# Top-32 attention with a routed feed-forward: selecting the last tile alone, a lighter mask, and earlier routing hops

## The chip, the cores and the metric

The kernel runs on one core of one Trainium2 chip. The metric is the device time of one execution in microseconds (us). TensorE (PE), VectorE (DVE), ScalarE (ACT), GpSimd (POOL) and SyncE (SP) each run their own instructions in order and meet through semaphores.

## The reference

Attention on q, k, v of 4 batches x 8 heads x 576 positions x 64, in which each query keeps only its 32 largest scores; the result, as 2304 tokens of 512 features, goes through a mixture of 8 experts with one expert for each token.

```
scores = q @ k.T / 8
kth    = 32nd largest of each row
attn   = softmax(where(scores >= kth, scores, -1e9))
x      = attn @ v                      # heads joined: 4 x 576 x 512
logits = x @ w_gate; local = sigmoid(x @ w_local)
e      = argmax(logits) if s == 0 or local < 0.5 else e of the token before
out    = softmax(logits)[e] * (relu(x @ w1[e]) @ w2[e])
```

## The kernel before

**Tiles and groups.** A unit is a pair of batches and a head; its 2 x 576 query rows make 9 tiles of 128 rows by 576 scores. All 16 units give 144 tiles. A round (`r`, 8 of them) handles two units in 6 groups (`k`) of 3 tiles (`j`). Rounds 1 to 3 are a hardware loop on each engine. Round 4 (`ROUND0`) is written out. Rounds 5 to 7 are written out on PE, ACT and POOL and are a hardware loop on DVE.

**The work on a group.** PE makes the scores of a tile and ACT copies them to `s_sb`, a ring of 9 slots (L760), two groups ahead. DVE finds the 32 largest in four passes of 8 (`largest`, L978 MAX8, L986 MATCH_REPLACE8 between the passes): 21 large instructions a group. The three tiles take turns, so that no instruction waits for the one just ahead. POOL then masks each tile in two passes: `(s < 32nd) * -1e9` into `p_sb` (L1277), and `p + s` (L1280). ACT takes the exponential and the row sum (L767), PE transposes (`turn`, L403), ACT copies the transposed tile (`take_pT`, L775), PE multiplies by v (`values`, L432), ACT copies (`take_oT`, L783), PE turns the group back and multiplies by the gate weights (`turn_back`, L444), ACT scales (`normalise`, L789, L797) and POOL adds the logits (`add_logits`, L1223, L1227). POOL also makes `nmax` (`biases`, L1261) and guards the row sums (`guard_sums`, L1216), which DVE inverts (`reciprocals`, L951).

**What sets the order.** Each engine's order is written out by hand. `step` on PE and ACT handles group `k`, with `values`, `take_oT` and `normalise` of the group before it; `ahead` makes the scores of the group after next. `slot` places parts of the early work at two places in a step.

**Early work.** After round 3 the first half of the tokens is complete. `early_routes` on PE and DVE works out, in hops placed in groups 1 to 4 of round 4, which token goes where. Then 29 parts (`early_parts`: a first transpose, and four parts for each of 7 row tiles) run one expert tile each for 7 experts, in slots of the following 19 groups; POOL gathers and scatters rows (`early_moves`).

**The last group.** After the loop DVE masks the three tiles itself (L1088, L1091), ACT takes three exponentials, and PE runs `turn`, `values(k-1)`, two `turn`s, `turn_back(k-1)`, `values`, `turn_back`. Then DVE routes the second half of the tokens (`choose`, L1005, and what follows), while PE fills its waits with the eighth early tile (`early_first`, L514; `early_second`, L522). PE's `code_rows` (L451) stand behind three quarters of one such product. The last stage, from 773 us on, is 15 expert tiles bound by PE (L681, L686).

## Time and profile before

| | us |
|---|---|
| median of 3 runs (lowest, highest) | 1013.66 (1013.32, 1015.21) |
| the profiled execution: its own time | 1011.88 |
| its span, first to last instruction | 1010.0 |
| busy: PE, DVE, ACT, POOL | 791.0, 762.0, 419.4, 613.7 |

Busy times are sums over the span; matmuls are pipelined, so a busy PE is not PE at its peak. The attention stage runs from about 20 to 747 us, the second routing to 773 us, the experts to the end. Line numbers are those of the kernel before.

### The profile page before, as it was taken

To read this page: it belongs to the slowest core of one execution; us is meant where nothing else is said; L and a number is where in the kernel's file an instruction comes from. 1 tells how busy PE (TensorE), PEld (TensorE's weight loads), DVE (VectorE), ACT (ScalarE), POOL (GpSimd) and SP (SyncE) were. 2 spreads that over 40 slices of the span, in tenths; PEclk is the share of its full clock that TensorE was granted. 3 is DMA by queue.
4 is the path that set the end of the run, shared out by engine and by line. 5 is a ranking of instruction groups with operands and counts; after the bars stand their busy time and mean duration, and the time that the engine had idled before them with its cause. 6 is when DMAs were issued, how large, how long until landed. Compare 5 with 4: busy or idle time off the path is not lost.

```text
span 1010.0 us, 16010 instructions
## 1 busy us (share of the span) xinstructions
PE 791.0 (78%) x3938; PEld 445.9 (44%) x3939; DVE 762.0 (75%) x1624; ACT 419.4 (42%) x914; POOL 613.7 (61%) x557
## 2 busy tenths in 40 slices
PE   2566666766766766567998889878888999999996
PEld 1343433434433443354554545545454444444442
DVE  5999999999999999899999999999944111111110
ACT  2445555544545555434565565656540111111111
POOL 0878887787878788568888888888812111101111
PEclk7667686676667577657999999999989999999998
DMA  3081001010101104010146145254135155454500
GB/s 122 1 352 65 20 31 49 2 48 13 36 13 35 48 0 142 1 48 22 60 178 235 55 183 219 81 205 184 57 146 188 51 190 208 189 195 162 232 22 27
DMA packets 17498, 103.98 MB, mean 103 GB/s; under 512 B 2638, under 2 KB 5198, under 8 KB 13328
## 3 DMA queue, kind: packets, MB, share of 16 engines
q1 hardware_dynamic: 10560, 57.68, 15.3%
q10 hardware_dynamic: 3024, 34.21, 8.6%
q0 software_dynamic: 3840, 11.28, 3.2%
q8 instruction: 25, 0.41, 0.2%
q14 instruction: 49, 0.40, 0.1%
HBM read 93.72 MB, written 10.75 MB: 103 GB/s over the span
## 4 chain that ended last, share of the span: by engine, by line
DVE 35%; PE 29%; issue 27%; POOL 3%; ACT 2%; DVEq 2%; DMA 1%; ACTq 0%; POOLq 0%
DVE top L978 19%; DVE work L986 13%; PE ps L681 10%; PE ps L686 10%; POOL p_sb L1277 2%; DVEq L200 2%; PE ps L522 1%; PE ps L403 1%; PE ps L670 1%; PE ps L432 1%; PE ps L514 1%; DMA wg_sb<-in_wg 1%; POOL p_sb L1280 1%; PE ps L662 1%; ACT p_sb L767 1%
## 5 line engine op out<-in xcount | busy, mean ns | idle before, releaser
L1277 POOL TENSOR_SCALAR p_sb<-s_sb,top 128x576 f32<-128x576 f32 x141 | 314.5, 2231 | 92.4 <-DVE top L978 89.2
L978 DVE MAX8 top<-work 128x8 f32<-128x576 f32 x432 | 302.4, 775 | 0.0
L403 PE MATMUL ps<-id_sb,p_sb 128*128 128x128 f32 x720 | 134.6, 331 | 184.6 <-ACT p_sb L767 184.6
L1280 POOL TENSOR_TENSOR p_sb<-p_sb,s_sb 128x576 f32<-128x576 f32 x141 | 198.6, 1409 | 26.2 <-POOL p_sb L1277 25.4
L986 DVE MATCH_REPLACE8 work<-top,work 128x576 f32<-128x576 f32 x288 | 213.8, 773 | 0.0
L403 PEld LDWEIGHTS ps<-id_sb,p_sb 128*128 128x128 f32 x720 | 99.0, 169 | 231.5 <-issue 231.5
L1174 DVE TENSOR_SCALAR moe<-ps 128x512 f32<-128x512 f32 x30 | 20.8, 692 | 193.3 <-PE ps L681 193.3
L393 PE MATMUL ps<-qk_sb 64*128 64x288 f32 (+1 forms) x640 | 140.5, 578 | 6.8 <-DMA qk_sb<-in_qk 5.9
L775 ACT ACTIVATE pT_sb<-ps 128x640 f32<-128x640 f32 x144 | 101.4, 704 | 104.7 <-PE ps L403 102.2
L767 ACT ACTIVATE p_sb<-p_sb,nmax 128x576 f32<-128x576 f32 x144 | 110.9, 770 | 79.4 <-POOL p_sb L1280 78.5
L432 PE MATMUL ps<-pT_sb,v_sb 128*64 128x64 f32 (+5 forms) x1152 | 123.5, 378 | 8.7 <-ACT pT_sb L775 8.7
L1331 POOL DMA_INDIRECT out<-moe,now_out x15 | 15.3, 1021 | 182.1 <-ACT moe L917 182.1
L681 PE MATMUL ps<-w_sb,moe 128*128 x240 | 108.1, 593 | 2.9 <-issue 2.9
L432 PEld LDWEIGHTS ps<-pT_sb,v_sb 128*64 128x64 f32 x1152 | 79.4, 173 | 69.7 <-issue 61.9
L686 PE MATMUL ps<-w_sb,moe 128*128 x240 | 108.0, 592 | 0.0
L760 ACT ACTIVATE s_sb<-ps 128x576 f32<-128x576 f32 x144 | 92.9, 646 | 34.0 <-PE ps L393 30.0
L986 DVE MATCH_REPLACE8 work<-top,s_sb 128x576 f32<-128x576 f32 x144 | 106.7, 770 | 0.0
L978 DVE MAX8 top<-s_sb 128x8 f32<-128x576 f32 x144 | 100.4, 770 | 7.0 <-POOL p_sb L1277 3.0
L910 ACT ACTIVATE moe<-ps 128x512 f32<-128x512 f32 x30 | 17.9, 597 | 131.3 <-PE ps L670 131.3
L393 PEld LDWEIGHTS ps<-qk_sb 64*128 64x128 f32 (+1 forms) x640 | 52.8, 219 | 40.6 <-issue 40.3
L681 PEld LDWEIGHTS ps<-w_sb,moe 128*128 128x128 f32 x240 | 44.3, 190 | 53.8 <-issue 53.8
L686 PEld LDWEIGHTS ps<-w_sb,moe 128*128 128x128 f32 x240 | 43.3, 190 | 43.0 <-issue 43.0
(155 smaller groups left out, 678.2 us busy)
## 6 DMA issues: line engine op xcount, KB each, us to landing
w_sb<-in_w SPq DMA_DIRECT2D x16, 2048.0 KB, 12.6
w_sb<-in_w ACTq DMA_DIRECT2D x16, 2048.0 KB, 10.6
qk_sb<-in_qk SPq DMA_DIRECT2D x16, 864.0 KB, 4.6
v_sb<-in_v SPq DMA_DIRECT2D x16, 320.0 KB, 2.9
x_dram<-x_sb SPq DMA_DIRECT2D x2, 1024.0 KB, 5.8
x_dram<-x_sb SPq DMA_DIRECT2D x2, 768.0 KB, 4.6
x_dram<-x_sb SPq DMA_DIRECT2D x2, 256.0 KB, 2.4
wg_sb<-in_wg ACTq DMA_DIRECT2D x1, 292.0 KB, 8.1
```

The source lines that it names most:

```text
L393: mm = pe.matmul(ps[o, bank + half, 0:HALF], qk_sb[d, a, two, q], qk_sb[d, a, two, S:S + HALF], start=True, stop=True)
L403: mm = pe.transpose(ps[:, bank + c // 4, (c % 4) * P:(c % 4 + 1) * P], p_at(n % GROUP)[:, c * P:(c + 1) * P], id_sb[:, :])
L432: mm = pe.matmul(ps[D * low:D * low + D, 4, q], v_sb[:, a, two, chunk, :], pT_sb[:, chunk, q], start=c == 0, stop=c == 2)
L681: return pe.matmul(ps[:, 1 + half, :], xT_sb[:, par, k, :], w1_sb[:, bass.ds(at1 + (k * F + half * 512), 512)], start=k == 0, stop=k == DC ...
L686: return pe.matmul(ps[:, 5 + par, :], hT_sb[:, f, :], w2_sb[:, bass.ds(at2 + f * MODEL, MODEL)], start=f == 0, stop=f == FC - 1)
L760: act.activation(s_at(n % RING).rearrange("p (h n) -> p h n", h=2), ps[:, bank:bank + 2, 0:HALF], ACT.Copy, scale=D ** -0.5).then_inc(evac, 1)
L767: act.activation(p_at(j)[:, 0:S], p_at(j)[:, 0:S], ACT.Exp, bias=nmax[:, k % 2, j:j + 1], accum_out=psum[:, k % 2, j:j + 1]).then_inc(p_do ...
L775: act.activation(pT_sb[:, :, j * P:(j + 1) * P], ps[:, bank:bank + 2, :].rearrange("p b (c q) -> p (b c) q", q=P)[:, 0:KC, :], ACT.Copy).t ...
L978: dve.max(top[:, par, j, rnd, :], src).then_inc(chain, 1)
L986: dve.match_replace(work[:, j, :], top[:, par, j, rnd, :], src, NEG).then_inc(chain, 1)
L1277: pool.tensor_scalar(p_at(j)[:, 0:S], s_at(n % RING), top[:, k % 2, j, ROUNDS - 1, 7:8], -BIG, ALU.is_lt, ALU.mult).then_inc(masked, 1)
L1280: pool.tensor_tensor(p_at(j)[:, 0:S], p_at(j)[:, 0:S], s_at(n % RING), ALU.add).then_inc(added, 1)
```

## The change

Four things are changed.

1. **Mask.** POOL makes `edge = 32nd * 2^100` of each tile (128x1), ACT computes `relu(edge - 2^100 * s)` into `p_sb` (`below`), which is 0 for scores kept and huge for the others, and POOL subtracts it from `s`. In `step` ACT runs `below` of tiles 0 and 1 right behind `ahead(k, 0)` and ahead of `take_oT`, and `below` of tile 2 behind `take_pT` of tile 0. DVE's wait for a free `top` buffer is on `edge_done` in place of `masked`.
2. **Last group.** DVE's round 7 is written out. Its last group (`last_group`) passes over tiles 0 and 1 first, and then over tile 2 alone, each instruction waiting for the one before. Tiles 0 and 1 are masked by ACT and POOL, tile 2 by DVE. ACT's and PE's order behind it is new.
3. **Early routing.** The hops of `early_routes` are placed earlier, the gathers too.
4. **Early parts.** The 29 parts are spread over 38 slots in place of 37, from one slot earlier on.

```
+            def below(r, n):
+                act.wait_ge(edge_done, BIAS + t + 1)
+                hold(act, turned, BIAS + t - GROUP + 1)
+                act.activation(p_at(j)[:, 0:S], s_at(n % RING), ACT.Relu, bias=edge[:, k % 2, j:j + 1],
+                               scale=-STEEP).then_inc(masked, 1)
 ACT step:
                     ahead(k, 0)
+                    below(r, GROUP * k)
+                    below(r, GROUP * k + 1)
                     take_oT(*before(r, k))
                     exponentiate(r, GROUP * k)
                     slot(r, k, 0)
                     take_pT(r, GROUP * k)
+                    below(r, GROUP * k + 2)
                     exponentiate(r, GROUP * k + 1)
 ACT behind the last step:
-            for j in range(GROUP):
+            for j in range(GROUP - 1):
+                below(r, GROUP * k + j)
+            take_oT(r, k - 1)
+            for j in range(GROUP - 1):
                 exponentiate(r, GROUP * k + j)
             take_pT(r, GROUP * k)
-            take_oT(r, k - 1)
+            normalise(r, k - 1)
             take_pT(r, GROUP * k + 1, 0)
+            exponentiate(r, GROUP * k + 2)
             take_pT(r, GROUP * k + 2)
-            normalise(r, k - 1)
 PE behind the last step:
+            values(r, k - 1)
             turn(r, GROUP * k)
-            values(r, k - 1)
+            turn_back(r, k - 1)
             turn(r, GROUP * k + 1, 0, 2)
+            values(r, k, range(GROUP - 1))
             turn(r, GROUP * k + 2, 2, 2)
-            turn_back(r, k - 1)
-            values(r, k, range(GROUP - 1))
             values(r, k, range(GROUP - 1, GROUP))
 DVE:
-            with dve.Fori(ROUND0 + 1, UNITS // 2) as r:
+            with dve.Fori(ROUND0 + 1, UNITS // 2 - 1) as r:
                 largest(r, False)
+            largest(UNITS // 2 - 1, False)
+            last_group()
 DVE last_group:
+                for j in range(GROUP):
+                    best(j, 0)
+                for rnd in range(ROUNDS - 1):
+                    for j in range(late):
+                        strike(j, rnd)
+                    for j in range(late):
+                        best(j, rnd + 1)
+                    if rnd == 0:
+                        reciprocals(g - 2, par)
+                strike(late, 0)
+                reciprocals(g - 1, 1 - par)
+                for rnd in range(1, ROUNDS):
+                    dve.wait_ge(chain, base + count[0])
+                    best(late, rnd)
+                    dve.wait_ge(chain, base + count[0])
+                    if rnd < ROUNDS - 1:
+                        strike(late, rnd)
+                dve.tensor_scalar(... -BIG, ALU.is_lt, ALU.mult).then_inc(last_masked, 1)
+                dve.wait_ge(added, BIAS + TILES - 1)
+                dve.tensor_tensor(..., ALU.add).then_inc(added, 1)
+                reciprocals(g, par)
 POOL mask, for each group:
+                    edges(0); guard_sums(k - 1); add_logits(k - 2); edges(1)
+                    subtract(0); edges(2); subtract(1); subtract(2)      # last group: no edges(2), no subtract(2)
+                    early_moves(...)                                     # first gathers at q == FROM - 1
 hops of early_routes:
-  PE (2, 1), (3, 0), (3, 1)              DVE (3, 2), (4, 0), (4, ROUNDS - 1)
+  PE (2, 0), (2, 1), (3, 0)              DVE (3, 0), (3, 2), (4, 1)
 early_parts:
-            at = [(q, j) for q in range(FROM, STEPS - 1) for j in range(SLOTS)][1:]
+            at = [(q, j) for q in range(FROM, STEPS - 1) for j in range(SLOTS)]
```

## Rows read from the trace of the kernel before

**Rows 1.** Windows: busy us (x instructions) of each engine, TensorE clock, DMA share, GB/s
```profile
590.00:643.00 53.00, 46.89 (x274) 27.28 (x271) 53.00 (x115) 32.45 (x72) 46.47 (x39) 1.00 0.33 126
```
**Rows 2.** Costliest groups: busy, mean ns of one | idle before, releaser
```profile
L1280 POOL TENSOR_TENSOR p_sb<-p_sb,s_sb 128x576 f32<-128x576 f32 x141 | 198.6, 1409 | 26.2 <-POOL p_sb L1277 25.4
L775 ACT ACTIVATE pT_sb<-ps 128x640 f32<-128x640 f32 x144 | 101.4, 704 | 104.7 <-PE ps L403 102.2
```
**Rows 3.** Timeline of DVE: start, us, operation [idle before <-releaser]; first MAX8 of four groups
```profile
276.31 2.08 DVE L978 MAX8 top<-s_sb 128x8 f32<-128x576 f32 x3 [1.71 <-ACT s_sb L760]
...
363.42 2.12 DVE L978 MAX8 top<-s_sb 128x8 f32<-128x576 f32 x3
...
645.12 2.08 DVE L978 MAX8 top<-s_sb 128x8 f32<-128x576 f32 x3 [1.47 <-POOL p_sb L1277]
704.14 2.08 DVE L978 MAX8 top<-s_sb 128x8 f32<-128x576 f32 x3 [0.48 <-ACT s_sb L760]
```
**Rows 4.** Timeline of all engines, first routing
```profile
407.54 2.22 POOL L1277 TENSOR_SCALAR p_sb<-s_sb,top 128x576 f32<-128x576 f32 x1 [3.25 <-DVE top L978]
...
411.43 0.24 POOL L1216 TENSOR_SCALAR psum_eps<-psum 128x3 f32<-128x3 f32 x1
411.44 0.78 ACT L767 ACTIVATE p_sb<-p_sb,nmax 128x576 f32<-128x576 f32 x1 [2.29 <-POOL p_sb L1280]
...
412.49 0.23 DVE L1026 TENSOR_REDUCE lsum<-lexp 128x9 f32<-128x72 f32 x1 [3.83 <-ACT lexp L833]
412.75 0.43 DVE L1027 TENSOR_SCALAR lsum<-lsum 128x9 f32<-128x9 f32 x1
...
415.29 2.13 DVE L1046 TENSOR_TENSOR_SCAN moe<-moe 64x576 f32<-64x576 f32 x1
417.46 0.82 DVE L1047 TENSOR_SCALAR moe<-moe,small_sb 64x576 f32<-64x576 f32 x1
```
**Rows 5.** Timeline of DVE, the same kinds of instruction in the second routing
```profile
750.71 1.36 DVE L1105 TENSOR_TENSOR_SCAN s_sb<-s_sb,ps 64x576 f32<-64x576 f32 x1 [1.20 <-ACT s_sb L894]
752.11 0.52 DVE L1108 TENSOR_SCALAR mine<-s_sb,small_sb 64x576 f32<-64x576 f32 x1
...
754.89 0.17 DVE L1027 TENSOR_SCALAR lsum<-lsum 128x9 f32<-128x9 f32 x1
```
**Rows 6.** Timeline of DVE, the last group and what follows it
```profile
718.67 2.07 DVE L978 MAX8 top<-s_sb 128x8 f32<-128x576 f32 x3
...
731.20 2.08 DVE L978 MAX8 top<-work 128x8 f32<-128x576 f32 x3
733.19 0.52 DVE L1088 TENSOR_SCALAR p_sb<-s_sb,top 128x576 f32<-128x576 f32 x1
733.74 0.76 DVE L1091 TENSOR_TENSOR p_sb<-p_sb,s_sb 128x576 f32<-128x576 f32 x1
...
747.86 0.23 DVE L1005 TENSOR_REDUCE lmax<-lg_all 128x9 f32<-128x72 f32 x1 [9.22 <-POOL lg_all L1227]
```
**Rows 7.** Timeline of PE around the last group, and one `turn_back` at the low clock
```profile
208.11 1.55 PE L444 MATMUL ps<-wg_sb,oT_sb 128*128 x6
...
727.33 0.71 PE L403 MATMUL ps<-id_sb,p_sb 128*128 128x128 f32 x5
...
735.61 1.30 PE L403 MATMUL ps<-id_sb,p_sb 128*128 128x128 f32 x5 [1.81 <-ACT p_sb L767]
736.84 3.47 PE L432 MATMUL ps<-pT_sb,v_sb 128*64 128x128 f32 x24
...
742.83 1.97 PE L432 MATMUL ps<-pT_sb,v_sb 128*64 128x256 f32 x36
745.55 0.86 PE L444 MATMUL ps<-wg_sb,oT_sb 128*128 128x73 f32 x6 [0.75 <-ACT oT_sb L783]
746.25 2.79 PE L514 MATMUL ps<-w_sb,moe 128*128 128x512 f32 x6
```
**Rows 8.** Windows, columns as in Rows 1
```profile
737.00:739.00 2.00, 2.00 (x18) 1.62 (x20) 0.21 (x2) 0.87 (x2) 0.22 (x1) 0.50 0.98 410
```

More of the change, by code:

```diff
@@ L65 @@
 BIG = 1e9
+STEEP = 2.0 ** 100
 EPS = 1e-9
@@ L96, in build @@
         nmax = sb("nmax", [P, 2, GROUP])
+        edge = sb("edge", [P, 2, GROUP])
         psum = sb("psum", [P, 2, GROUP])
@@ L213, in build @@
         masked = sem("masked")
+        edge_done = sem("edge_done")
+        last_masked = sem("last_masked")
         added = sem("added")
@@ L464, in early_routes @@
                     code_rows(1, 6, 0).then_inc(early_code_ps, 1)
-                elif (k, j) == (2, 1):
+                elif (k, j) == (2, 0):
                     count = early_rows[0]
@@ L469, in early_routes @@
                               start=True, stop=True).then_inc(early_base_ps, 1)
-                elif (k, j) == (3, 0):
+                elif (k, j) == (2, 1):
                     row = early_rows[2]
@@ L481, in early_routes @@
                     mm.then_inc(early_place_ps, 1)
-                elif (k, j) == (3, 1):
+                elif (k, j) == (3, 0):
                     pe.wait_ge(early_marked, 2)
@@ L751, in _ @@
             act.sem_inc(p_done, BIAS)
+            act.sem_inc(masked, BIAS)
             act.sem_inc(hT_done, BIAS)
@@ L963, in largest @@
                 for k in range(GROUPS):
+                    if isinstance(r, int) and GROUPS * r + k == TILES // GROUP - 1:
+                        break
                     base = CHAIN * (GROUPS * r + k)
@@ L967, in largest @@
                     n = 0
-                    hold(dve, masked, BIAS + t0 - GROUP)
+                    hold(dve, edge_done, BIAS + t0 - GROUP)
                     for rnd in range(ROUNDS):
@@ L1204, in _ @@
         def _(pool):
-            pool.sem_inc(masked, BIAS)
+            pool.sem_inc(edge_done, BIAS)
             pool.sem_inc(added, BIAS)
@@ L1243, in early_moves @@
             def early_moves(q):
-                if q == FROM:
+                if q == FROM - 1:
                     pool.wait_ge(early_row_in, 1)
@@ L1267, in mask @@
                 for k in range(GROUPS):
-                    base = CHAIN * (GROUPS * r + k)
-                    final = last and k == GROUPS - 1
-                    for j in range(GROUP):
-                        n = GROUP * k + j
-                        t = 2 * TPU * r + n
-                        if not final:
-                            hold(pool, turned, BIAS + t - GROUP + 1)
-                            hold(pool, chain, base + CHAIN - GROUP + j + 1)
-                            pool.tensor_scalar(p_at(j)[:, 0:S], s_at(n % RING), top[:, k % 2, j, ROUNDS - 1, 7:8], -BIG,
-                                               ALU.is_lt, ALU.mult).then_inc(masked, 1)
-                            hold(pool, masked, BIAS + t + 1)
-                            pool.tensor_tensor(p_at(j)[:, 0:S], p_at(j)[:, 0:S], s_at(n % RING),
-                                               ALU.add).then_inc(added, 1)
-                        if j == 0:
-                            if k > 0 or not first:
-                                guard_sums(*before(r, k, 1))
-                            if k > 1 or not first:
-                                add_logits(*before(r, k, 2))
-                            if isinstance(r, int) and r >= ROUND0:
-                                early_moves(GROUPS * (r - ROUND0) + k)
@@ new lines, in mask, with edges @@
+                    t0 = 2 * TPU * r + GROUP * k
+                    def edges(j):
+                        done = CHAIN - GROUP
+                        if isinstance(r, int) and GROUPS * r + k == TILES // GROUP - 1:
+                            done = GROUP + (GROUP - 1) * (2 * ROUNDS - 3)
+                        hold(pool, chain, CHAIN * (GROUPS * r + k) + done + j + 1)
+                        if not isinstance(r, int) or GROUPS * r + k > 1:
+                            hold(pool, masked, BIAS + t0 - 2 * GROUP + j + 1)
+                        pool.tensor_scalar(edge[:, k % 2, j:j + 1], top[:, k % 2, j, ROUNDS - 1, 7:8], STEEP, None,
+                                           ALU.mult).then_inc(edge_done, 1)
@@ new lines, in subtract @@
+                    def subtract(j):
+                        hold(pool, masked, BIAS + t0 + j + 1)
+                        pool.tensor_tensor(p_at(j)[:, 0:S], s_at((GROUP * k + j) % RING), p_at(j)[:, 0:S],
+                                           ALU.subtract).then_inc(added, 1)
+                    final = last and k == GROUPS - 1
+                    edges(0)
+                    if k > 0 or not first:
+                        guard_sums(*before(r, k, 1))
+                    if k > 1 or not first:
+                        add_logits(*before(r, k, 2))
@@ L1289, in mask @@
+                    edges(1)
+                    subtract(0)
+                    if not final:
+                        edges(2)
+                    subtract(1)
+                    if not final:
+                        subtract(2)
+                    if isinstance(r, int) and r >= ROUND0:
+                        early_moves(GROUPS * (r - ROUND0) + k)
                     if k < GROUPS - 1:
```

39 lines of the change are left out of this document (25 added, 14 removed).

## The prediction

> **What bounds the kernel now.** I read the windows first, then the waits of DVE and its timeline, then the timelines of all engines around the last group. In the attention stage DVE is busy for all of a 53 us window, with PE at 46.89, POOL at 46.47 and ACT at 32.45 [rows 1]: DVE sets the pace, 14.5 us a group (645.12 plus 5 groups is 718.67 less small gaps [rows 3, 6]). What happens on POOL and ACT inside a group costs nothing unless it makes DVE wait. DVE's waits between 20 and 718 us are few: about 1.5 us at each turn of its loop (two of the four are in [rows 3], the others lie between them), 0.48 us at 704.14 for scores [rows 3], and 3.83 us in the first routing for the exponentials of the logits [rows 4]. Leaving a loop costs nothing: the first group after it, at 363.42, has no idle time ahead [rows 3]. The second place that sets the time is the tail of the attention stage. DVE's last selection starts at 731.20 and takes 2.08 us; `choose` starts at 747.86 [rows 6]. Between them lie masks, exponentials, transposes and products, in a chain over four engines. Behind `choose` comes the second routing (25.4 us) and then the experts on PE; neither is changed, so what moves `choose` moves the end.
>
> **The sum is made against the profiled execution,** 1011.88 us with a span of 1010.0. That is 1.78 us below the median of the runs, 1013.66, so I take the differences from the profile and put them on the median.
>
> **1. The loop turn.** DVE's loop over rounds 5 to 7 becomes one over 5 and 6. One turn of the three goes, the last, 1.47 us [rows 3], and the exit that takes its place costs nothing by the row at 363.42. Bounds: 0, if the gap comes back as code loading, and 1.71, the largest gap. I take 1.47.
>
> **2. The lighter mask.** Removed on POOL: for 141 tiles a pass of 2.22 us [rows 4]; the one of 1.41 us stays, as a subtraction [rows 2]. Added on POOL: one 128x1 operation a tile. The small ones take 0.24 us [rows 4], so POOL falls from 12.7 us a group (46.47 of 53 us [rows 1]) by 3 x (2.22 - 0.24) to about 6.8. Added on ACT: one 128x576 pass a tile; no such Relu is in the trace, so between a pT copy (0.70 [rows 2]) and an exponential (0.78 [rows 4]) I take 0.7. Three a group, 2.1 us, bring ACT from 8.9 (32.45 of 53 us) to 11.0 of 14.5 us. DVE's pace hides both. What it costs if that cover is gone: `below` of tile 1 waits for DVE's last pass with `take_oT` and `exponentiate` queued behind it on ACT, and PE's `turn` behind those. The exponential of tile 0 comes about 2 us after DVE ends the group (edge 0.24, three small operations, edge 0.24, subtraction 1.41), where POOL's 3.64 us pair stood before, and that of tile 2 is no longer paced by three pairs. So the scores are copied earlier, and the 0.48 us wait at 704.14 should go (bounds 0 and 0.48; I take 0.48). PE has 46.89 of 53 us to do here, so a new wait on PE of more than 1.6 us a group would reach DVE; I see none.
>
> **3. The first routing's stall.** DVE waits for ACT's `lexp`, behind the exponential of tile 0 at 411.44, behind POOL's pair that started at 407.54 [rows 4]. After: edge at 407.55, `guard_sums`, `add_logits` and the second edge in steps of 0.3 to 0.4 to 409.2, subtraction to 410.7, exponential at 410.85. Gain 0.59 (bounds 0, and 1.9, if the small operations cost nothing).
>
> **4. DVE beside POOL.** In that stretch the scan takes 2.13 us, the comparison 0.82 and the small TENSOR_SCALAR 0.43 [rows 4], where the same kinds take 1.36, 0.52 and 0.17 in the second routing, with POOL idle [rows 5]. The excess is 0.77 + 0.30 + 0.26 = 1.33. After, POOL has no work there beyond the second subtraction: `below` of tile 2 stands behind `take_pT`, which waits for PE, which now waits in slot (2, 0) for this very routing. I take 1.1 (bounds 0 and 1.33). A rule of the Trainium skill bears on this (SBUF — State Buffer, the section on what contends): DVE and GpSimd share one pair of SBUF ports as a lock held for a whole instruction, against DVE operations with two SBUF inputs or in a two-port mode. The rows agree with it; by it alone the gain would be at most the same 1.33. It speaks against the change at one place: DVE's own mask of the last tile would start behind POOL's second subtraction. That would be some 0.6 us, and it would lie in the slack shown under 6.
>
> **5. The earlier hops.** PE waits in slot (2, 0) to about 419, with `turn` of that group behind it (it ran at 412.45 before). That holds the group's transposes up by some 7 us; DVE needs the scores made in this step by about 434, and the rest of the step is some 8 us of work. The hops of DVE move among its passes and find their inputs ready. The gathers hold POOL for some 2 us behind its masks, with `biases` behind them, whose result is wanted 5 us later. I take 0 for all of it, and for the spread of the parts over 38 slots (the last part stays in its slot); bounds: a loss of 2, if PE's late transposes reach DVE's next scores, and a gain of 0.3.
>
> **6. The tail.** Count from the start of DVE's last group, 718.67 before; `choose` is at +29.2 [rows 6]. DVE: 15 large instructions and then 6 alone, of about 0.79 each with their wait, so tile 2 is selected at +15.3 in place of +14.6, and masked (0.52 + 0.76 [rows 6]) at +16.6. That was the path before; now ACT and PE are later than it, and the 0.7 us cost nothing. Tiles 0 and 1 are selected by +9.8 and +10.5. Their masks stand on ACT behind the whole step of the group before. In that step PE has two halves of an early product, and the transpose of tile 0 comes at about +4.6 (+8.7 before: 727.33 [rows 7]), tile 2's at +10.4, its copy is done at +11.9. Then `values(k-1)`: 24 matmuls, 3.47 us at the low clock, half of it at the high one [rows 7, 8]. From here the clock decides. Before, a transpose at 727.33 took 0.71 us, at the high clock, and one at 735.61 took 1.30, at the low one; PE had done little but three transposes between. It was low through `values(k-1)` and high again for the values at 742.83 [rows 7, 8]. Now PE thins out 3 to 4 us sooner, so I expect the low clock (0.50, 1.2 GHz) from about +9 on. Then: values to +15.4; `take_oT`; exponentials at +16.0 and +16.8; `turn` at +17.0 (1.30 [rows 7]); `turn_back(k-1)` 1.55 [rows 7], `turn` 1.30 to +21.1; pT copy and the third exponential to +22.7, behind the +16.6 of its mask by 5 us. If the clock is high again from +22 on: `values` of two tiles 1.3 (of the 1.97 for all three [rows 7]) to +23.3, `turn` 0.71, copy 0.70 to +24.9, the last values to +25.7, oT to +26.4, `turn_back` at +26.5, and 2.31 us from there to `choose` (745.55 to 747.86 [rows 6, 7]): +28.8. The tail gains 0.4. With the high clock throughout it comes to about +25.3, a gain of 3.9; with the low one throughout to +31.6, a loss of 2.4, and more behind it (below). I take 0.4: before, the clock came back behind `values` and transposes without a gap between them, and the new order offers the like of that only from +12 on.
>
> **The sum:** 1.47 + 0.48 + 0.59 + 1.1 + 0 + 0.4 = 4.0. On the median: 1009.6 (1007.9 for a profiled execution like this one).
>
> **Rivals.**
> *A. The clock stays low to the end of the tail.* For it: in the new order PE waits between transposes and products several times, for `take_pT` and for `take_oT`, where PE ran `values` and the turns behind them without a gap before. Against it: the clock came back behind just these products. Place: from `values` of tiles 0 and 1 on. Price: 2.4 us later at `choose`; and PE's six matmuls of 512 columns, 2.79 us at the high clock [rows 7], take 5.5 from +30.2 and hold `code_rows` to +35.7, where DVE's codes are ready at +33.2: 2.5 more. Loss 4.9 against the 3.6 of terms 1 to 4: 1.3 slower, 1015.0. It decides from the point at which `choose` and the wait of `code_rows` together come 3.6 us later than before. This is the case on the other side.
> *B. The clock is high from the first products on.* For it: the transpose at +8.7 was at the high clock before [rows 7]. Against it: the thinner PE. Then 3.6 + 3.9 = 7.5: 1006.2.
> *C. The attention stage gives nothing:* the loop gap returns as code loading for the written-out round, and the late step in the first routing eats terms 3 and 4. For it: the only written-out round on DVE is the one that ran on from 363.42 [rows 3], so one example carries term 1, and no row shows PE waiting in slot (2, 0). Against it: that one example had no gap. Only 0.48 and 0.4 are left: 1012.8.
>
> **How the numbers follow.** Forecast 0.42, A 0.25, B 0.18, C 0.15. What a measurement can tell from no change is 0.2%, about 2 us. Faster by more: the forecast but for a tenth or so, B, and none of C: 0.57. Within: the rest of the forecast, most of C, half of A: 0.30. Slower: the other half of A with little from the terms before: 0.13. The range from B's edge to A's: 1005.8 to 1014.9.
>
> **What would show it.** DVE: three loop turns with a gap in place of four, none at the last round; no wait for scores in the last round; the first routing's wait near 3.2 us and its scan near 1.4; `choose` 4 us sooner. Windows of 1 us over the last 30 us of the stage: the clock 0.50 from about 10 us after the last group's start. PE: the last three `turn`s at 1.3, 1.3 and 0.7. Wrong would be a wait on DVE in rounds 5 to 7, DVE waiting for `psum_eps` inside the last group, a third exponential that starts right at the end of its mask, or a `code_rows` that starts well after DVE's codes.

## The result: slower by 0.34%, where 0.4% faster was forecast

| | before | after |
|---|---|---|
| median of all runs, us | 1015.27 (20 runs, 1011.09 to 1017.7) | 1018.72 (20 runs, 1014.87 to 1021.48) |
| ratio, 95% interval | | 1.0034 (1.0023 to 1.0046) |
| profiled execution, span, us | 1011.88, 1010.0 | 1018.89, 1017.1 |
| mean granted clock | 0.849 | 0.834 |
| busy PE, DVE, ACT, POOL, us | 791.0, 762.0, 419.4, 613.7 | 811.4, 760.2, 514.5, 332.1 |
| last group starts | 718.67 | 720.01 |
| `choose`, `code_rows` | 747.86, 749.43 | 753.06, 755.87 |

The medians differ by 3.45 us, the two profiled executions by 7.01: the one of before lies 3.4 below its median and that of after on its own. So the terms below, which add up to 7, are some twice what the medians show. They say where these two executions differ; what the kernels differ by is told by the ratios. How much one execution can add shows in e4, e5 and e6 (below): up to the last group they are the kernel after, instruction for instruction, and their last groups start at 717.75, 716.82 and 717.51, not at 720.01. The mean granted clock says the same: over its 20 executions after has 0.839 (0.833 to 0.846), and before has 0.843 to 0.846 in the means of its five sets of runs, so the trace of after, at 0.834, lies near its lowest and that of before, at 0.849, above its mean.

POOL lost 282 us of work, as the edit says, and ACT gained 95. Before, two passes a tile stood on POOL [rows 2, 4]; now POOL has one and ACT one. From the page of after, one of its costliest groups (busy, mean ns | idle before it):

```profile
L1339 POOL TENSOR_TENSOR p_sb<-s_sb,p_sb 128x576 f32<-128x576 f32 x143 | 201.8, 1412 | 167.2 <-ACT p_sb L773 127.8
```

POOL now waits 127.8 us for ACT's new pass (L773). DVE's waits in after (total us, times, longest):

```profile
...
DVE rinv L970 <- POOL psum_eps L1273: 9.8, 2, 5.4
DVE top L999 <- ACT s_sb L765: 6.2, 7, 1.6
...
DVE lsum L1094 <- ACT lexp L846: 3.2, 1, 3.2
...
```

Seven times DVE waited for ACT to bring scores, 6.2 us in all, and an eighth time, 0.4 us, in the last group (L1022), where I had forecast the one wait of 0.48 [rows 3] gone. One of the eight, 1.59 us at 554.05, is the turn of DVE's loop; 5.0 us are left. Its timeline shows where (first MAX8 of four groups):

```profile
554.05 2.08 DVE L999 MAX8 top<-s_sb 128x8 f32<-128x576 f32 x3 [1.59 <-ACT s_sb L765]
...
643.20 2.08 DVE L999 MAX8 top<-s_sb 128x8 f32<-128x576 f32 x3 [0.99 <-ACT s_sb L765]
...
704.98 2.08 DVE L999 MAX8 top<-s_sb 128x8 f32<-128x576 f32 x3 [1.14 <-ACT s_sb L765]
...
720.01 2.08 DVE L1022 MAX8 top<-s_sb 128x8 f32<-128x576 f32 x3 [0.40 <-ACT s_sb L765]
```

At the start of round 6 after is ahead (554.05 against 556.10). The first group of that round takes 15.0 us (14.8 before), the next three to 612.59 the 14.52 of before. The seven from there to the last take 15.0 to 15.8, and it is 1.34 late at the last group. The ledger up to `code_rows`: -2.05 to round 6, +3.39 to the last group, +3.86 in the tail, the time from the last group's start to `choose` (33.05 in place of 29.19), +1.24 between `choose` and `code_rows`: +6.44 of the 7.01. The rest lies in the stage behind, which no run changes and which took 260.6 us before, 261.2 after, and between 260.3 (e4) and 263.1 (e13) elsewhere. Windows over the same stretch, first after, then before (us, busy PE, PEld, DVE, ACT, POOL, TensorE clock, DMA share, GB/s):

```profile
590.00:717.00 127.00, 110.84 (x625) 64.83 (x623) 122.36 (x262) 87.38 (x182) 52.84 (x86) 0.93 0.37 137
```
```profile
590.00:717.00 127.00, 111.62 (x664) 65.25 (x661) 124.93 (x268) 75.26 (x166) 109.46 (x92) 0.99 0.38 143
```

DVE was idle for 2.6 us more, PE did less work (625 records in place of 664) in nearly the same busy time, at a clock of 0.93 in place of 0.99, and ACT and POOL were both far from full. So no engine became the bound by its own load. What did is a chain of two engines. PE's first transpose of a step shows it falling behind in after:

```profile
572.96 0.74 PE L407 MATMUL ps<-id_sb,p_sb 128*128 128x128 f32 x5 [1.79 <-ACT p_sb L780]
...
606.20 0.71 PE L407 MATMUL ps<-id_sb,p_sb 128*128 128x128 f32 x5
```

It starts 3.9 us after DVE's group at 569.03, 8.1 after that at 598.07, and 9.6 to 10.4 after the starts of the seven long ones and of the last group; there the scores of that step come too late, and DVE goes at PE's pace. Inside two steps of PE, after first, before second (the first row of each step is its first transpose):

```profile
683.82 0.71 PE L407 MATMUL ps<-id_sb,p_sb 128*128 128x128 f32 x5
...
699.59 0.71 PE L407 MATMUL ps<-id_sb,p_sb 128*128 128x128 f32 x5
...
702.65 0.74 PE L407 MATMUL ps<-id_sb,p_sb 128*128 128x128 f32 x5 [0.86 <-ACT p_sb L780]
...
705.73 0.73 PE L407 MATMUL ps<-id_sb,p_sb 128*128 128x128 f32 x5 [1.66 <-ACT p_sb L780]
...
707.35 3.53 PE L436 MATMUL ps<-pT_sb,v_sb 128*64 128x256 f32 x36 [0.20 <-ACT pT_sb L788]
...
714.74 0.71 PE L407 MATMUL ps<-id_sb,p_sb 128*128 128x128 f32 x5
```
```profile
684.30 0.71 PE L403 MATMUL ps<-id_sb,p_sb 128*128 128x128 f32 x5
...
699.40 0.71 PE L403 MATMUL ps<-id_sb,p_sb 128*128 128x128 f32 x5
...
701.81 0.74 PE L403 MATMUL ps<-id_sb,p_sb 128*128 128x128 f32 x5 [0.19 <-ACT p_sb L767]
...
704.89 0.74 PE L403 MATMUL ps<-id_sb,p_sb 128*128 128x128 f32 x5 [1.65 <-ACT p_sb L767]
...
706.51 1.97 PE L432 MATMUL ps<-pT_sb,v_sb 128*64 128x256 f32 x36 [0.20 <-ACT pT_sb L775]
...
712.35 0.71 PE L403 MATMUL ps<-id_sb,p_sb 128*128 128x128 f32 x5
```

The wait of PE's second transpose grew from 0.19 to 0.86 us, by 0.67 (3.06 from the first in place of 2.41), and the 36 products behind the third took 3.53 us, at the low clock (1.2 GHz), in place of 1.97. In after that happened at every second group from 615 on (3.51, 3.32, 3.47, 3.53); before, in its one trace, all of these took 1.84 to 1.97 up to the tail.

The first transposes give PE's real allowance. In this stretch the steps go in pairs, one with two early products and one with a single one. Before they took 15.10 and 12.95 us (684.30, 699.40, 712.35), 28.05 together, where DVE's two groups take 29.04: 1.0 us was free, 0.5 a group. After they took 15.77 and 15.15, 30.92 together. Of the 2.87 more, twice 0.67 is the longer wait, and 1.56 the low clock.

ACT in that place:

```profile
700.39 0.70 ACT L788 ACTIVATE pT_sb<-ps 128x640 f32<-128x640 f32 x1
700.99 0.77 ACT L773 ACTIVATE p_sb<-s_sb,edge 128x576 f32<-128x576 f32 x1
701.66 0.76 ACT L780 ACTIVATE p_sb<-p_sb,nmax 128x576 f32<-128x576 f32 x1
```

The new pass of tile 2 (`below`, 700.99) stands between the copy of tile 0's transposes and the exponential of tile 1, for which PE waits; it moves that exponential by 0.67 us.

### The profile page after: what moved, and what is told of

It is laid out like the page before. It is cut to its first block, busy times and chain, and to the rows that moved or that the text cites. A ratio compares the mean times of both kernels' runs of the same rounds, so it can differ in the third digit from the quotient of the medians.

```text
span 1017.1 us, 16220 instructions
## 1 busy us (share of the span) xinstructions
PE 811.4 (80%) x3938; PEld 460.5 (45%) x3939; DVE 760.2 (75%) x1620; ACT 514.5 (51%) x1057; POOL 332.1 (33%) x561
## 4 chain that ended last, share of the span: by engine, by line
PE 33%; DVE 31%; issue 25%; ACT 4%; DMA 3%; DVEq 2%; POOL 1%; ACTq 0%; POOLq 0%; SPq 0%
DVE top L999 17%; DVE work L1007 12%; PE ps L685 10%; PE ps L690 9%; PE ps L518 3%; PE ps L526 3%; PE ps L436 3%; PE ps L407 2%; ACT p_sb L780 2%; DMA w_sb<-in_w 1%; DVEq L202 1%; ACT pT_sb L788 1%; PE ps L674 1%; DMA wg_sb<-in_wg 1%; PE ps L666 1%
## 5 line engine op out<-in xcount | busy, mean ns | idle before, releaser
L999 DVE MAX8 top<-work 128x8 f32<-128x576 f32 x423 | 292.2, 748 | 0.0
L1339 POOL TENSOR_TENSOR p_sb<-s_sb,p_sb 128x576 f32<-128x576 f32 x143 | 201.8, 1412 | 167.2 <-ACT p_sb L773 127.8
L1007 DVE MATCH_REPLACE8 work<-top,work 128x576 f32<-128x576 f32 x282 | 206.7, 745 | 0.0
L407 PEld LDWEIGHTS ps<-id_sb,p_sb 128*128 128x128 f32 x720 | 102.6, 174 | 206.9 <-issue 206.5
L1231 DVE TENSOR_SCALAR moe<-ps 128x512 f32<-128x512 f32 x30 | 20.7, 692 | 194.0 <-PE ps L685 194.0
L397 PE MATMUL ps<-qk_sb 64*128 64x288 f32 (+1 forms) x640 | 144.0, 589 | 6.8 <-DMA qk_sb<-in_qk 6.0
L436 PE MATMUL ps<-pT_sb,v_sb 128*64 128x64 f32 (+5 forms) x1152 | 129.4, 390 | 9.3 <-ACT pT_sb L788 9.3
L773 ACT ACTIVATE p_sb<-s_sb,edge 128x576 f32<-128x576 f32 x143 | 108.2, 770 | 46.6 <-POOL edge L1334 46.5
L436 PEld LDWEIGHTS ps<-pT_sb,v_sb 128*64 128x64 f32 x1152 | 82.7, 178 | 71.4 <-issue 64.2
L1334 POOL TENSOR_SCALAR edge<-top 128x1 f32<-128x1 f32 x143 | 30.5, 213 | 237.0 <-DVE top L999 228.1
L1399 POOL DMA_INDIRECT out<-moe,now_out x15 | 15.3, 1017 | 182.8 <-ACT moe L936 182.8
L685 PEld LDWEIGHTS ps<-w_sb,moe 128*128 128x128 f32 x240 | 44.3, 190 | 54.5 <-issue 54.4
```

The lines of the kernel that those rows point to most:

```text
L397: mm = pe.matmul(ps[o, bank + half, 0:HALF], qk_sb[d, a, two, q], qk_sb[d, a, two, S:S + HALF], start=True, stop=True)
L407: mm = pe.transpose(ps[:, bank + c // 4, (c % 4) * P:(c % 4 + 1) * P], p_at(n % GROUP)[:, c * P:(c + 1) * P], id_sb[:, :])
L436: mm = pe.matmul(ps[D * low:D * low + D, 4, q], v_sb[:, a, two, chunk, :], pT_sb[:, chunk, q], start=c == 0, stop=c == 2)
L685: return pe.matmul(ps[:, 1 + half, :], xT_sb[:, par, k, :], w1_sb[:, bass.ds(at1 + (k * F + half * 512), 512)], start=k == 0, stop=k == DC ...
L773: act.activation(p_at(j)[:, 0:S], s_at(n % RING), ACT.Relu, bias=edge[:, k % 2, j:j + 1], scale=-STEEP).then_inc(masked, 1)
L999: dve.max(top[:, par, j, rnd, :], src).then_inc(chain, 1)
```

## The experiments

Ratios are to the kernel before, run beside each, with 95% intervals.

### Which part costs

**e7_mask_alone**: before with the lighter mask only. **e9_mask_moves_last**: the same with the gathers behind the subtractions.

```diff
-  bias, then add        (two POOL passes a tile)
+  edge, subtract        (POOL)   + below   (ACT)
   # e9 also: early_moves(...) behind subtract(2)
```


> The kernel before with the lighter mask alone: edge on GpSimd, below on ScalarE, subtract on GpSimd, in the places of the changed kernel; hops, parts, loop and tail are those of before. Theory S: VectorE waits for scores in the last two rounds as in the changed kernel (5 us or more in all), its last group starts 2 to 4 us later than before, and the time is 2 to 4 us over the kernel before. Rival: the mask costs nothing in the steady stage (last group within 1 us of 718.7), and the changed kernel's loss is the tail's alone.

> The kernel of e7 (the lighter mask alone) with early_moves on GpSimd behind the three subtractions, as in the changed kernel, and not between the edges of tiles 0 and 1. In e7 VectorE waited 4.7 us once for an edge that stood behind a scatter. Theory: that was an artefact of e7, worth 3.2 us; without it the mask alone costs 2 to 3.5 us against the kernel before (1.002 to 1.0035), as waits for scores in the last two rounds. Rival: the mask's cost stays at 5 us or more.

Measured 1.0052 (1.0035 to 1.0069) and 1.0048 (1.0035 to 1.0062); tails of 31.13 and 31.12 us. One 4.7 us wait in e7, for an `edge` queued behind a scatter on POOL, made me doubt it; without that queue the ratio stayed. The 2 to 3.5 us expected of e9 was too little: the mask, with its ACT pass where the change puts it, costs some 5 us by itself.

**e2_round_written_out**, **e3_hops_alone** and **e8_hops_and_round** (both):

```diff
-  with dve.Fori(ROUND0 + 1, UNITS // 2) as r: largest(r, False)
+  with dve.Fori(ROUND0 + 1, UNITS // 2 - 1) as r: largest(r, False)
+  largest(UNITS // 2 - 1, False)
```


> The kernel before with VectorE's last round written out, nothing else. Term 1 of the prediction: one turn of the loop, 1.47 us, goes: ratio 0.9985. Rival: VectorE is not alone in setting the pace in the last rounds (TensorE is as late as the scores it owes), the gap comes back as a wait for scores: ratio 1.000, with VectorE's waits for scores up by the same 1.5 us.

> The kernel before with the earlier routing hops, the gathers one group earlier behind the three masks, and the parts over 38 slots. The step chain's theory: within 1 us of the kernel before. Rival P: the new spread puts more full steps one behind the other around groups 9 to 13 and costs 2 us or more, to be seen as VectorE's waits for scores from 600 us on.

> The kernel before with the earlier hops, the spread of the parts and VectorE's last round written out; mask and tail as before. If the two add, last group's start is 1.4 us before that of the hops alone (716.99), at 715.6, and the time 2 to 3 us under the kernel before (0.997 to 0.998). If TensorE's lateness takes the place of the loop's turn, the two together give no more than either: 0.999.

0.9992 (0.9976 to 1.0008), 0.999 (0.9973 to 1.0007), and together 0.9969 (0.9947 to 0.9991). In e2 the gap of 1.47 at round 7 is gone, and scores are late by 1.4 us in 3 waits; in e3 DVE waits for no scores from 590 on. Together they give 0.3%, clear of noise; either alone is not, and whether the two add or help each other the intervals don't tell.

**e4_old_tail**: after, with the last group, its orders and DVE masks as before. This is mask, hops and round without the new tail.


> The changed kernel with the old tail: VectorE selects the last group's three tiles in turn and masks them, ScalarE and TensorE have their old order behind the last step. If the new tail gains what it is for (its own part, from the start of the last group to choose), this kernel is 1 to 3 us slower than the changed one. Rival T: the new tail costs, and this one is 2 to 4 us faster. By the traces (last group to choose: 29.2 us before, 33.1 after, of which the lateness of TensorE explains 1.7) I expect it 1 to 2 us faster than the changed kernel.

0.9995 (0.9977 to 1.0013), 0.4% (some 4 us) below after where 1 to 2 us were expected; tail 31.17. So mask +0.48%, hops and round -0.31%, tail +0.39%: +0.56% added up, +0.34% measured; the first three give -0.05% in e4 in place of +0.17%. That difference of 0.22% is inside the intervals, so no interplay of the parts is shown.

### Why the mask costs

**e1_below2_later** and **e10_later_old_tail** (with e4's tail): the pass behind `exponentiate(1)`. **e13_below2_hidden** and **e14_hidden_old_tail**: behind `exponentiate(0)`, where ACT next waits for PE.

```diff
   exponentiate(r, GROUP * k)
+  below(r, GROUP * k + 2)      # e13, e14
   slot(r, k, 0)
   take_pT(r, GROUP * k)
-  below(r, GROUP * k + 2)
   exponentiate(r, GROUP * k + 1)
+  below(r, GROUP * k + 2)      # e1, e10
```


> The changed kernel with one line moved: below of tile 2 stands behind exponentiate of tile 1 on ScalarE, not ahead of it. Theory S (the step chain): that pass, 0.67 us, delays the exponential of tile 1 and with it TensorE's second turn in every group, TensorE's thinner work also drops its clock more often, and from about 600 us on TensorE is behind VectorE. Then the wait of TensorE before the second turn goes back from 0.86 to about 0.2 us where the slots are full, VectorE's waits for scores in the last rounds (6.2 us in 7 waits) fall under 1.5, and the time falls by 4 to 6 us against the changed kernel, to 0.1% to 0.3% under the kernel before. Rival T (the tail alone, its new orders and VectorE's 5.4 us wait for psum_eps): the waits for scores go but the time falls by under 2 us. Rival P (the spread of the parts): no change within 1 us.

> The changed kernel with both repairs: below of tile 2 behind the exponential of tile 1 (e1) and the old tail (e4). If the two causes add, it is 4.5 + 1.8 us faster than the changed kernel, 1012 to 1013, ratio 0.998 of before. If the place of below counts for nothing beside the tail, it equals e4 (0.9995).

> The changed kernel with below of tile 2 right behind the exponential of tile 0, ahead of slot(k, 0), where ScalarE waits some 2 us for TensorE. Theory S: the pass costs only where it stands between two answers that TensorE waits for; here TensorE's wait before the second turn goes back to 0.2 us with no new wait before the scores, VectorE's waits for scores in rounds 6 and 7 fall from 6.6 to under 2 us, and the time falls by 3 to 4 us against the changed kernel (1.0005 of before). Rival (ScalarE's load or the two passes of tiles 0 and 1 ahead of take_oT): no better than e1 (1.0025).

> e13 with the old tail. If TensorE's lateness is gone, the last group starts at 714 to 716, the tail is 29.2 to 30, and the time is under e4's (0.9995) by 2 to 3 us: 0.997. Rival as for e13: like e4 and e10, 0.9995 to 1.0002.

e1: 1.0025 (1.001 to 1.004); e10: 1.0002 (0.9988 to 1.0017). One place later gains nothing that can be told, where 4 to 6 us (e1) and 0.998 (e10; e4 has 0.9995) were expected: PE's second transpose waits 0.19 again, but now scores and their copies wait. PE in e10, one row of the new wait:

```profile
704.86 0.76 PE L397 MATMUL ps<-qk_sb 64*128 64x288 f32 x4 [0.47 <-ACT s_sb L765]
```

e13: 0.9971 (0.9955 to 0.9987); e14: 0.9964 (0.9948 to 0.998). Against after that is 0.6%, by moving one ACT pass. From 570 us on DVE's groups are all 14.52 us and it waits for no scores; tails 30.8 and 29.02. PE in e13, same place of the group as above:

```profile
698.38 0.74 PE L407 MATMUL ps<-id_sb,p_sb 128*128 128x128 f32 x5 [0.19 <-ACT p_sb L780]
...
701.46 0.74 PE L407 MATMUL ps<-id_sb,p_sb 128*128 128x128 f32 x5 [1.65 <-ACT p_sb L780]
...
703.08 1.97 PE L436 MATMUL ps<-pT_sb,v_sb 128*64 128x256 f32 x36 [0.20 <-ACT pT_sb L788]
```

The waits are those of before. The clock is that of before in this place, but not in the whole stretch: at 615 and 673 the products took over 3.4, at 645 2.3. ACT's pass is the same 0.76 us, only ahead of a wait of ACT's own:

```profile
706.78 0.76 ACT L773 ACTIVATE p_sb<-s_sb,edge 128x576 f32<-128x576 f32 x1
...
709.12 0.60 ACT L822 ACTIVATE moe<-ps 128x512 f32<-128x512 f32 x1 [1.10 <-PE ps L518]
```

**e11_filled** and **e16_filled_less**: is it the wait or the clock? The pass stays where the change has it, and PE gets matmuls on constants, whose results nobody reads, ahead of its waits in rounds 5 to 7: 4 and 4 in e11, 1 and 2 in e16 (the second only where no early product fills the slot).

```diff
   hold(pe, pT_done, BIAS + t - slots + 1)
+  for _ in range(filled):
+      pe.matmul(ps[:, 3, 256:512], id_sb[:, :], wg_sb[:, 0:256], start=True, stop=True)
   hold(pe, p_done, BIAS + t + 1)
```


> The changed kernel with idle work on TensorE in rounds 5 to 7: four matmuls of 128x256 into an unused part of PSUM before the second turn, and before the third where its slot is empty, while TensorE waits for the exponential (some 0.9 us in a wait of 1 to 1.5). They compute nothing that is used. Theory S with the clock: the 0.67 us pass alone is small, the low clock that the thinner work brings (values of 3.5 us in place of 2.0 at 707 us) makes up the most of the loss; filled, the clock stays at 1.00 in the last rounds, VectorE's waits for scores fall from 6.6 under 3 us, and the time falls by 2 to 4 us. Rival: the clock is not the cause; the filled kernel is the same or slower by up to 1 us.

> e11 with less filling: one matmul of 128x256 (0.49 us) in the wait of 0.86 before the second turn, two (0.97) in the wait of 1.66 before the third where its slot is empty. Clock theory: the clock in rounds 6 and 7 is 1.00 in place of 0.93, no values of 3.5 us, waits for scores under 3 us, and the time 2 to 3 us under the changed kernel. Rival: TensorE's own late work, not the clock, is the bound, and the time is within 1 us of the changed kernel or above it.

e11: 1.0094 (1.0061 to 1.0128): four of them took 1.94 us, not the 0.9 I had sized them at, and DVE waited 18.8 us for scores in 11 waits. It decides nothing on the clock, but says what PE's slack is: less than this. e16: 0.9974 (0.9955 to 0.9993), 0.6% below after. PE in e16:

```profile
695.84 0.71 PE L409 MATMUL ps<-id_sb,p_sb 128*128 128x128 f32 x5
...
697.89 0.64 PE L406 MATMUL ps<-wg_sb,id_sb 128*128 128x256 f32 x2
698.91 0.74 PE L409 MATMUL ps<-id_sb,p_sb 128*128 128x128 f32 x5 [0.38 <-ACT p_sb L783]
...
703.61 1.97 PE L438 MATMUL ps<-pT_sb,v_sb 128*64 128x256 f32 x36 [0.20 <-ACT pT_sb L791]
```

and its window, to be read against the two above:

```profile
590.00:717.00 127.00, 118.58 (x687) 68.64 (x687) 125.02 (x265) 93.30 (x196) 56.56 (x93) 1.00 0.37 137
```

PE does 7.7 us more in the stretch than in after and the kernel is faster. The second transpose is as late as in after (3.07 us from the first), but the clock is 1.00, the products took 1.84 to 1.97 in every step, and DVE waits 1.9 us for scores in 2 waits. A pair of steps takes 29.38 us (680.06 to 709.44), a third of a microsecond over DVE's 29.04. The trace is of e16's second slowest execution, 1016.12; over its twelve the mean clock is 0.852. In the last step the matmuls ran at the low clock, one pair of them in 2.05 us, and the tail of this trace is 34.74 us, so they pay in the steps and not there.

What the traces say of the clock, each by one execution (clock from 590 to 717 us; DVE's waits for scores in rounds 6 and 7, the loop turn aside):

| kernels | place of tile 2's pass | clock | waits for scores, us |
|---|---|---|---|
| e3, e8, e12 | none, old mask | 0.95, 0.97, 0.96 | 0 |
| before, e2 | none, old mask | 0.99, 0.95 | 0.5, 1.1 |
| e13, e14 | hidden | 0.96, 0.95 | 0 |
| e15, e17, e18 | hidden, DVE without loops | 0.97 | 0.8, 0.8, 0 |
| e1, e10 | one place later | 0.95, 0.92 | 2.3, 6.0 |
| e4, e5, e6, e9 | as in the change | 0.96 | 3.5, 2.8, 3.2, 3.3 |
| e7 | as in the change | 0.94 | 6.7 |
| after | as in the change | 0.93 | 5.0 |
| e16 | as in the change | 1.00 | 1.9 |

So the low clock does not come from the pass. It is there without the lighter mask (in e3 the products at 615.30 took 3.63 us and DVE waited for nothing), and hiding the pass doesn't lift it: 0.96 in e13 as in e4, and over all executions 0.837 in e13 against 0.839 in after. At nearly one clock, 0.95 to 0.96, the place of the pass makes the difference between 3 us of waits and none. Given the pass in that place, the waits grow as the clock falls: 1.9 us at 1.00, 3 at 0.96, 5.0 at 0.93 (e7, with its wait behind a scatter, stands a little off). The Trainium skill (TensorE: Matmul & The Clock Gate, "Loop structure matters more than you think") says that the loop nest decides whether matmuls keep the fast clock. The rows agree in that matmuls put ahead of PE's waits took the clock of the stretch to 1.00 (e16); the place of one ACT pass did not move it.

### The tail

**e5_oT_behind**: `take_oT(k-1)` behind the two exponentials. **e6_reciprocal_later**: DVE's `reciprocals(g-1)`, which waits for POOL inside the last group, behind the last tile's selection.

```diff
-  take_oT(r, k - 1)                          # e5 (ACT)
   for j in range(GROUP - 1): exponentiate(r, GROUP * k + j)
+  take_oT(r, k - 1)
   strike(late, 0)                            # e6 (DVE, last_group)
-  reciprocals(g - 1, 1 - par)
   for rnd in range(1, ROUNDS): ...
+  reciprocals(g - 1, 1 - par)
```


> The changed kernel with take_oT of the last group but one behind the two exponentials, not ahead of them. Theory S2 (the tail's path runs through values(k-1), take_oT, exponential, turn): the exponential of tile 0 starts at the end of its subtraction, under values(k-1), and the first turn follows values(k-1) within 0.2 us, not 1.5. The tail, last group to choose, falls from 33.1 by 1.0 to 1.5 us, and the time by as much or up to 2.5 where the clock holds. Rival T (VectorE's wait for psum_eps): the same as the changed kernel.

> The changed kernel with VectorE's reciprocal of the last group but one behind the selection of the last tile, so that its 5.4 us wait for psum_eps doesn't hold the selection up. S2: the wait goes or stands behind the selection, the mask of tile 2 is done 4 to 5 us sooner, and the tail stays at 33 within 0.5 us, because the third exponential stands behind take_pT of tile 1 on ScalarE. Rival T: the tail and the time fall by 3 us or more.

The tail of after, PE:

```profile
730.39 0.71 PE L407 MATMUL ps<-id_sb,p_sb 128*128 128x128 f32 x5
...
736.22 1.30 PE L407 MATMUL ps<-id_sb,p_sb 128*128 128x128 f32 x5 [1.64 <-ACT p_sb L780]
738.40 3.28 PE L436 MATMUL ps<-pT_sb,v_sb 128*64 128x128 f32 x24 [0.89 <-ACT pT_sb L788]
743.17 0.74 PE L407 MATMUL ps<-id_sb,p_sb 128*128 128x128 f32 x5 [1.49 <-ACT p_sb L780]
...
744.37 0.71 PE L407 MATMUL ps<-id_sb,p_sb 128*128 128x128 f32 x5
746.25 1.30 PE L436 MATMUL ps<-pT_sb,v_sb 128*64 128x256 f32 x12 [1.17 <-ACT pT_sb L788]
747.48 0.77 PE L407 MATMUL ps<-id_sb,p_sb 128*128 128x128 f32 x5
749.13 0.89 PE L436 MATMUL ps<-pT_sb,v_sb 128*64 128x64 f32 x24 [0.89 <-ACT pT_sb L788]
750.76 0.86 PE L448 MATMUL ps<-wg_sb,oT_sb 128*128 128x73 f32 x6 [0.74 <-ACT oT_sb L796]
751.46 4.48 PE L518 MATMUL ps<-w_sb,moe 128*128 128x512 f32 x6
755.87 0.41 PE L455 MATMUL ps<-idb_sb,carry 128*32 128x128 bf16 x7
```

`values(k-1)` ends 21.7 us after the last group's start, as before (+21.6 [rows 7]). Then before ran turns and values without a wait and had `turn_back` at +26.9; after waits 1.49, 1.17 and 0.89, and has it at +30.8. All the 3.9 us are lost there. By cause they are two things: the new order costs 1.8 to 1.9 us (33.05 against 31.17 in e4, 30.8 in e13 against 29.02 in e14), and the place of the pass 2.1 to 2.3 (31.17 against 29.02, 33.05 against 30.8). e5: 1.0016 (1.0002 to 1.0031), 0.2% below after, which the intervals just don't separate; its tail is 32.74, 0.3 us shorter where 1.0 to 1.5 was expected. The 1.49 is gone, 0.84 for oT comes back, and the six products ahead of `code_rows` run at the high clock:

```profile
738.56 0.77 PE L407 MATMUL ps<-id_sb,p_sb 128*128 128x128 f32 x5
740.17 0.86 PE L448 MATMUL ps<-wg_sb,oT_sb 128*128 128x73 f32 x6 [0.84 <-ACT oT_sb L796]
...
747.96 2.79 PE L518 MATMUL ps<-w_sb,moe 128*128 128x512 f32 x6
751.13 0.41 PE L455 MATMUL ps<-idb_sb,carry 128*32 128x128 bf16 x7 [0.38 <-DVE code L1084]
```

e6: 1.0039 (1.002 to 1.0057), no gain. DVE's wait, 5.44 us in after, is the eye-catching row of that stretch:

```profile
736.63 0.18 DVE L970 RECIPROCAL rinv<-psum_eps 128x3 f32<-128x3 f32 x1 [5.44 <-POOL psum_eps L1273]
...
740.80 1.40 DVE L1052 TENSOR_SCALAR p_sb<-s_sb,top 128x576 f32<-128x576 f32 x1
742.30 0.76 DVE L1056 TENSOR_TENSOR p_sb<-p_sb,s_sb 128x576 f32<-128x576 f32 x1
```

In e6 1.34 us of it are left, and the last tile is selected 15.3 us after the group's start in place of 20.7. The mask of tile 2 is done only 0.4 us sooner (+22.7 in place of +23.1), since DVE's addition now waits 3.82 us for POOL's subtractions, and the tail is 33.19 in place of 33.05. So e6 did not bring the mask forward by the 4 to 5 us expected. That DVE is not on the path is read from the rows of after: ACT starts the third exponential at 745.98, right behind a pT copy and 2.9 us after that mask is done. The wait for `psum_eps` was one of my signs of failure, and it costs nothing.

### What could be had

**e12_no_loop_on_dve**: e8 with every DVE round written out. **e15_hidden_no_loop**: e14 with the same. **e17_routing_spared**: e15, with the pass back behind `take_pT` in the one step of the first routing, since e13 lost term 3 there. **e18_new_tail_repaired**: e17 with the new tail and e5's order.

```diff
-  with dve.Fori(...) as r: largest(r, False)   # the loops of rounds 1-3 and 5-6
+  for r in range(1, UNITS // 2): largest(r, False)
```


> The kernel of e8 (old mask and tail, earlier hops) with all of VectorE's rounds written out. If a turn of the loop costs 1.5 us wherever it stands, three more go, and the time falls by 4.4 us against e8, to 0.9925 to 0.994 of before. If TensorE's lateness takes their place, it is like e8 (0.997).

> e14 with all of VectorE's rounds written out: e12 with the lighter mask in the hidden place. The mask's own gain, 1.7 to 1.9 us in the first routing, should show now: 1003.5 to 1004.5, 0.990 of before. Rival: the mask costs more than that in TensorE's steps, and this one is 1 to 3 us over e12 (0.9918).

> e15 with below of tile 2 back behind take_pT in the one step of the first routing. Group 2 of round 4 takes 25.3 us again, and the time falls by 1.5 to 2 us against e15, to 1004, at or under e12 (0.9918). Rival: the 2 us come back as a wait for scores one or two groups later, like e15.

> e17 with the changed kernel's tail and take_oT behind the two exponentials. If the path behind values(k-1) is what the new tail lengthens, it stays 0.5 to 1.5 us longer than the old one even so (30 us against 29): the time is 0 to 2 us over e17. Rival: with TensorE on time the last tile selected alone pays, and it is 1 us or more under e17.

| | ratio (95%) | median | last group | tail |
|---|---|---|---|---|
| e12 | 0.9918 (0.9896 to 0.994) | 1005.46 | 710.64 | 29.78 |
| e15 | 0.9932 (0.9906 to 0.9958) | 1006.17 | 711.34 | 29.01 |
| e17 | 0.9907 (0.9882 to 0.9931) | 1004.54 | 710.12 | 29.16 |
| e18 | 0.9922 (0.99 to 0.9944) | 1006.43 | 709.3 | 27.88 |

Written-out rounds bring 0.5% from e8 to e12 and 0.3% from e14 to e15. e15 was expected at 0.990 and is no better than e12. In e17 the routing's group took 26.4 us, between the 25.3 expected and e15's 27.4. e17 beats both kernels, by 0.9% and 1.3%; it is not told apart from e12, which has the old mask. The lighter mask, well placed, is worth nothing that shows here (e14 against e8: 0.9964 and 0.9969). The same goes for the new tail once PE's step is repaired: in its profile it is 1.3 us shorter (27.88), its time is not.

## Why the prediction was wrong

**Term 2 failed, and with it the start of term 6.** It read: "PE has 46.89 of 53 us to do here, so a new wait on PE of more than 1.6 us a group would reach DVE; I see none." Both halves were wrong. There was a new wait, of 0.67 us a group, because I placed `below` in ACT's total of 2.1 us a group and not in its order: between two links for which PE waits in turn. And 1.6 us was no allowance. It took the idle share of PE for slack, while that idle time is the waits of a chain of PE and ACT (1.65 and 0.19 of it in the rows above). A pair of steps took 28.05 of the 29.04 us that DVE needs for two groups, so the allowance was 0.5 us a group, and 0.67 is over it. The low clock takes from the same allowance, 1.56 us in the values of a pair; the sum has no term for it before the tail. With the old mask that was bearable: slow products at 615, 645 and 674 us led to no wait (e3). With the pass as well it was not. e7 and e9 refute "DVE's pace hides both" (+0.5%), and e13, which moves nothing but the pass, shows the first half of the cause: 0.6%. The second half, how much the clock adds to it, rests on single traces and on e16, where added matmuls and the clock of 1.00 come together. The 0.48 us of scores, which was to go, became 5.0.

**Term 6** had the right path (ACT and PE, not DVE) from a wrong start. I put the first transpose of the last step, which belongs to the group before, at +4.6; it came at +10.4, later even than before (+8.7), since the step came late into the group. Tile 2's was forecast at +10.4 and came at 736.22, +16.2; the end of `values(k-1)` at +15.4, came at +21.7. The clock was low later than I had it: 1.00 until +14, 0.50 from +15 to +21.6 (forecast from +9), 1.00 until +31. From the last group's first `turn` to `choose` I had 11.8 us and it took 9.9, with that turn at 0.74 and not 1.30: the clock came back sooner than I forecast, and that softened a 6 us error to 4.2. With the pass hidden the same new tail took 30.8 (e13), 1.8 us more than the old one (29.02 in e14), where I had it 0.4 shorter.

**Rival A** had the right sign for the wrong reason, and that its price came out was luck. Its second half came true in small: the six products took 4.48 in place of 2.79 us and `code_rows` came 2.81 us behind `choose`, in place of 1.57 [rows 6, 7, and 749.43]. Its first did not; after +22 the transposes were at 0.71 to 0.77. Its price of 4.9 was nearly met (3.86 + 1.24 = 5.1), by the new order and the place of the pass. Its time had the gains of terms 1 to 4 in full, and they did not come in full. The slow six products are no mark of the new tail either: it ran them in 2.79 in e5, e13 and e18.

**Term 1** held: no gap for code at round 7, and every further turn removed pays too (e12). In after the row at 643.20 still has 0.99 of idle time, for scores. **Terms 3 and 4** held nearly: DVE's first-routing group took 25.24 us in place of 27.14, a gain of 1.9 where 0.59 + 1.1 was forecast. After, in that place:

```profile
411.68 0.23 DVE L1094 TENSOR_REDUCE lsum<-lexp 128x9 f32<-128x72 f32 x1 [3.16 <-ACT lexp L846]
411.94 0.39 DVE L1095 TENSOR_SCALAR lsum<-lsum 128x9 f32<-128x9 f32 x1
...
414.44 1.35 DVE L1114 TENSOR_TENSOR_SCAN moe<-moe 64x576 f32<-64x576 f32 x1
415.83 0.51 DVE L1115 TENSOR_SCALAR moe<-moe,small_sb 64x576 f32<-64x576 f32 x1
```

The wait fell from 3.83 to 3.16, the scan from 2.13 to 1.35, the comparison from 0.82 to 0.51 [rows 4]; the small TENSOR_SCALAR, from 0.43 to 0.39, hardly did. DVE's own mask of the last tile started beside POOL's subtraction and took 0.9 us more than alone, where term 4 had 0.6, in the slack as forecast. **Term 5** held: the moved hops cost nothing (e3, 0.999). In sum, after led by 2.05 us at round 6; the steps from there gave back 3.4, net of term 1, and the tail and `code_rows` 5.1.

**Open.** Why the clock falls at every second group of after, and not at the same places in each execution: no run has the low clock at will, and e16 adds work as well as clock. Whether the new tail of e18 is worth anything. What exactly a loop turn on DVE spends.

## What to carry to other kernels

An engine's idle share is not slack where it waits in turn with another engine: before adding work to an engine that is busy for 61% of the time, as ACT was [rows 1], find the waits of the engines that it answers, measure what their steps take from start to start, and put the work where it waits itself, not between two answers (0.6% here for one line). Leave room for the granted clock: its low stretches came with and without the change, and took 1.56 us of a pair that had 1.0 to spare. And test the largest idle row before believing it: 5.4 us on DVE were free, 0.67 us on PE were not.

## What the hardware showed that I had not expected

- Each DVE loop turn costs 1.4 to 1.7 us and writing the rounds out removes it: 1010.58 to 1006.17 us (e14, e15).
- 0.64 us of useless matmuls ahead of one wait and 1.10 ahead of another went with a clock of 1.00 from 590 to 717 us (0.93 in after) and a kernel faster by 0.6% than after (e16).
- A DVE TENSOR_SCALAR of 128x576 took 1.40 us beside POOL's subtraction and 0.52 alone (e6, and [rows 6]). POOL's pair took 2.77 us at 739.11, no longer than elsewhere, so DVE alone was held. The Trainium skill (SBUF — State Buffer, "Who interferes with whom") says that where DVE works in a two-port mode, whoever issues first gets the shared ports for the whole instruction and the other is blocked; the rows agree, since DVE's 740.80 plus 1.40 ends 0.3 us behind POOL's end at 741.88.
- An fp32 matmul of 128x256 takes 1.94 / 4 = 0.49 us at the high clock, in two records (e11).
